# A fused attention and two-MoE kernel: order of the copies of means, the queue of the first V, and the step at which weight loads begin

## The reference, cut to what matters

```python
def _attn_ref(q, k, v):                     # B=2, H=8, S=768, D=64
    block, window = (32, 16)
    k_sum = k.reshape(B, H, nb, block, D).max(axis=3)
    v_sum = v.reshape(B, H, nb, block, D).mean(axis=3)
    scores_l = scale * q @ k^T              # kept where |i - j| < window
    scores_s = scale * q @ k_sum^T + log(block)
    a = softmax(concat[scores_l_m, scores_s])
    return a @ concat[v, v_sum]
x = transpose(attn_out).reshape(B, S, 512)
h = relu(x @ w_in);  gate = sigmoid(conv3(h, conv_w));  x = (h * gate) @ w_out
x + relu(layernorm(x) * g_ln @ w_ch1) @ w_ch2
```

## Time and profile before

| | before |
|---|---|
| median of 3 runs | 472.86 us (471.78 to 473.08) |
| profiled execution | 473.34 us, of which the span 471.60 us |
| busy: TensorE / VectorE / ScalarE / GpSimd | 457.3 / 279.9 / 200.7 / 265.9 us |
| mean granted TensorE clock | 0.996 of full speed |
| attention, steps up to 19 | until about 72 us |
| data moved by DMA | 33.61 MB in 61702 packets, 44608 of them under 512 bytes |

### The profile page before, as it was taken

The page is one execution under the profiler, slowest core; times in us unless marked ns, Lnnn a source line. Parts: engine busy times, 40 slices in busy tenths (PEclk is TensorE's granted clock), DMA queues, the critical chain, the costliest instruction groups (busy, mean ns, idle before and its releaser), DMA issues.

```text
span 471.6 us, 8651 instructions
## 1 busy us (share of the span) xinstructions
PE 457.3 (97%) x3143; PEld 404.1 (86%) x3143; DVE 279.9 (59%) x625; ACT 200.7 (43%) x499; POOL 265.9 (56%) x409
## 2 busy tenths in 40 slices
PE   6889899999999999999999999999999999999997
PEld 6667678999898998989899888989998989899985
DVE  4878896787665886894655534466652334243333
ACT  3977798533335657435423342423410331233110
POOL 3636789999905000067988778790014488788100
PEclk9998999999999999999999999999999999999999
DMA  9998872121101100001122102211020102220003
GB/s 210 195 223 201 195 182 59 46 90 45 46 0 31 60 0 1 1 0 44 47 90 89 59 33 90 89 46 44 1 111 24 61 30 89 90 72 20 0 1 133
DMA packets 61702, 33.61 MB, mean 71 GB/s; under 512 B 44608, under 2 KB 55900, under 8 KB 61660
## 3 DMA queue, kind: packets, MB, share of 16 engines
q1 hardware_dynamic: 60092, 32.66, 24.6%
q10 hardware_dynamic: 1568, 0.39, 0.4%
HBM read 28.72 MB, written 3.15 MB: 68 GB/s over the span
## 4 chain that ended last, share of the span: by engine, by line
PE 86%; SPq 8%; DVE 2%; DMA 1%; issue 1%; POOL 0%; ACT 0%; DVEq 0%; POOLq 0%
PE two L1454 9%; PE two L1455 9%; PE two L1453 9%; PE two L1430 8%; PE two L1433 8%; PE two L1432 8%; PE two L1279 5%; PE two L1281 5%; PE two L1280 5%; PE two L1359 5%; PE two L1360 5%; PE two L1358 5%; SPq L381 2%; SPq L370 2%; SPq L391 1%; PE two L1264 1%
## 5 line engine op out<-in xcount | busy, mean ns | idle before, releaser
L1430 PE MATMUL two<-combo,wa 128*128 128x384 f32 x224 | 75.9, 339 | 0.0
L1455 PE MATMUL two<-wv,h 128*128 128x512 f32 x192 | 75.4, 393 | 0.0
L1433 PE MATMUL two<-combo,wa 128*128 128x384 f32 x224 | 75.4, 336 | 0.0
L1454 PE MATMUL two<-wv,h 128*128 128x512 f32 x192 | 75.3, 392 | 0.0
L1432 PE MATMUL two<-combo,wa 128*128 128x384 f32 x224 | 75.2, 336 | 0.0
L1453 PE MATMUL two<-wv,h 128*128 128x512 f32 x192 | 75.0, 391 | 0.0
L569 POOL TENSOR_TENSOR asum<-wst 128x256 f32<-128x256 f32 x26 | 22.3, 858 | 92.4 <-PE two L1281 50.2
L598 POOL TENSOR_TENSOR wa<-wst,wa 128x256 fp32r<-128x256 f32 x39 | 29.6, 786 | 36.6 <-ACT wa L1059 36.6
L532 POOL TENSOR_SCALAR pn<-ex,rinv 128x120 f32<-128x120 f32 x96 | 33.2, 364 | 22.5 <-DVE rinv L659 22.5
L563 POOL TENSOR_TENSOR wa<-asum,wa 128x256 fp32r<-128x256 f32 x52 | 43.5, 836 | 4.3
L1279 PE MATMUL two<-xT,win 128*128 128x384 f32 x128 | 43.5, 340 | 0.0
(11 more groups left out here) (114 smaller groups left out, 984.5 us busy)
## 6 DMA issues: line engine op xcount, KB each, us to landing
wst<-in_moe_w_ch SPq DMA_DIRECT2D x26, 512.0 KB, 3.3
vW<-in_v SPq DMA_DIRECT2D x16, 240.0 KB
kn<-in_k SPq DMA_DIRECT2D x15, 192.0 KB, 3.6
qn<-in_q SPq DMA_DIRECT2D x15, 192.0 KB, 3.4
out<-y SPq DMA_DIRECT2D x11, 256.0 KB, 2.0
wst<-in_moe_w_in SPq DMA_DIRECT2D x8, 256.0 KB, 3.4
wst<-in_moe_w_out SPq DMA_DIRECT2D x8, 256.0 KB, 3.1
vW<-vs SPq DMA_DIRECT2D x16, 72.0 KB
```

The lines of the kernel that those rows point to most:

```text
L1430: nc.tensor.matmul(o, wk[:, 0, kk], ck[:, 0, kk], start=(first and kk == 0), stop=False, skip_group_check=True)
L1433: ins = nc.tensor.matmul(o, wk[:, 1, kk], ck[:, 0, kk], start=False, stop=(kk == 1), skip_group_check=True)
L1454: nc.tensor.matmul(o, hi, vl, start=False, stop=False, skip_group_check=True)
L1455: ins = nc.tensor.matmul(o, lo, vh, start=False, stop=(f == NFP - 1 and c == 1), skip_group_check=True)
```

## The change

1. SyncE no longer issues V of pair 0. ScalarE does, right after its two first loads and before its first copy of queries.
2. SyncE issues Q of pair 1 and K of pair 2 right after K of pair 1, and from pair 2 on the copies of means (`load_vsum(p)`) ahead of `load_q(p + 2)`.
3. VectorE copies the means of pair p + 1 at the end of the second step of pair p instead of in the third, and doesn't wait for outputs of step 3p any more. In exchange TensorE waits before outputs of step 3p (pairs 1 to 6) until that copy is done.
4. TensorE transposes keys of pair p + 2 before outputs of step 3p instead of after them. Scores of step 7, their maxima and their exponentials come earlier.
5. Weight splits start in step 14 instead of 9; the loads are issued at pairs 4, 5 and 6 instead of 2, 3, 5 and 6.

```diff
-        SPLIT_STEP = 9
+        SPLIT_STEP = 14
...
+        def v_parts(p):
+            b, hp = p // PPB, p % PPB
+            hh = v[b, 2 * hp:2 * hp + 2]
+            dst = vW[p % 3][:].rearrange("p n (h d) -> p n h d", h=2)
+            return [(dst[0:KEYS, 1:NQ - 1, 0], v_windows(b, 2 * hp, 1, NQ - 2, 0, KEYS)),
+                    (dst[0:KEYS, 1:NQ - 1, 1], v_windows(b, 2 * hp + 1, 1, NQ - 2, 0, KEYS)),
+                    (dst[WIN:KEYS, 0], hh[:, 0:KEYS - WIN].rearrange("h p d -> p h d")),
+                    (dst[0:KEYS - WIN, NQ - 1], hh[:, S - KEYS + WIN:S].rearrange("h p d -> p h d"))]
...
             load_k(1)
-
-            sp.wait_ge(pool_init, 1)
-            load_v(0)
             load_q(1)
             load_k(2)
+
+            sp.wait_ge(pool_init, 1)
             load_v(1)
...
+                load_vsum(p)
                 if p + 2 < NPAIR:
                     load_q(p + 2)
-                load_vsum(p)
-                for n in {2: (0,), 3: (1,), 5: (2,), 6: (3,)}.get(p, ()):
+                for n in {4: (0,), 5: (1,), 6: (2,)}.get(p, ()):
                     load_w(n)
...
-            for n in range(4, 8):
+            for n in range(3, 8):
                 load_w(n)
...
                 if p >= 2:
-                    dve.wait_ge(o_ready, GPP * (p - 1) + 1)
                     dve.wait_ge(v_in[(p - 2) % 3], v_loads(p - 2))
...
             row_sums(5)
+            score_max(7)
+            x_low(1)
             key_max(3)
+            means_out(2)
             window_keys(3)
-            x_low(1)
-            means_out(2)
...
                     row_sums(n)
+                    if p + 1 < NPAIR:
+                        means_out(p + 1)
                 elif p + 1 < NPAIR:
-                    means_out(p + 1)
                     row_sums(n)
...
             nc.scalar.dma_start(qn[:, 0, :, 1], q[0, 1].rearrange("(t p) d -> p t d", p=P)).then_inc(qn_in[0], 16)
+            act.wait_ge(pool_init, 1)
+            for dst, src in v_parts(0):
+                nc.scalar.dma_start(dst, src).then_inc(v_in[0], 16)
             queries(0, (slice(0, GB), slice(GB, NQ)))
...
+                if n % GPP == 0 and 3 <= n < GPP * (NPAIR - 1):
+                    pe.wait_ge(vm_done, p + 2)
...
             probs_t(3)
+            scores(7)
             keys_t(3)
...
                 if t == 1 and p + 1 < NPAIR:
                     block_means(p + 1)
+                    if p + 2 < NPAIR:
+                        keys_t(p + 2)
...
                 outputs(n - 1)
-                if t == 1 and p + 2 < NPAIR:
-                    keys_t(p + 2)
```

More of the change, by code:

```diff
@@ L376, in load_v @@
                     sp.wait_ge(o_ready, GPP * (p - 2))
[L377 to L384, removed]
+                for dst, src in v_parts(p):
+                    sp.dma_start(dst, src).then_inc(v_in[p % 3], 16)
             def load_vsum(p):
@@ L728, in _ @@
             row_sums(5)
+            score_max(7)
+            x_low(1)
             key_max(3)
+            means_out(2)
             window_keys(3)
-            x_low(1)
-            means_out(2)
             for n in range(6, NG):
                 p, t = n // GPP, n % GPP
-                if n + 1 < NG:
+                if 6 < n < NG - 1:
                     score_max(n + 1)
@@ L984, in _ @@
                 p, t = n // GPP, n % GPP
-                exps(n)
+                if n != 7:
+                    exps(n)
                 if n == 6:
@@ L988, in _ @@
                     x_high(2)
+                    exps(7)
                 elif t == 0:
@@ L1320, in _ @@
                     queries_t(p + 1)
-                if n + 2 < NG:
+                if 7 < n + 2 < NG:
                     scores(n + 2)
```

## The result

| | before | after |
|---|---|---|
| median, same chip, 20 executions each | 472.41 us (471.61 to 474.93) | 470.75 us (468.68 to 473.28) |
| ratio after to before | | 0.9951, 95% interval 0.9931 to 0.9972 |
| profiled execution, and its span | 473.34, 471.60 us | 470.99, 469.27 us |
| first probabilities of steps 6, 9, 12, 15, 20 | 28.02, 38.72, 47.07, 57.20, 71.73 | 28.34, 36.20, 44.53, 52.80, 69.78 |

The change makes the kernel 0.5% faster, 1.7 us by the medians and 2.3 by the ratio. The executions of the new kernel fall into two groups: nine lie between 468.68 and 469.33 us, eight between 471.09 and 473.28, three at 470.56 to 470.99. Six tenths of a per cent lie between the two groups of one and the same program, and the profiled execution, 470.99, is in the middle.

The account below looks back on a forecast made before the run. SyncE's gapless queue of issues was taken to bound the attention stage. The terms 0.4 + 4.88 - 0.6 = 4.7 us, off the median of 472.86, gave 468.2 us, with a range of 465.9 to 471.3.

Parts of the forecast that it names:

- What bounds the kernel: Attention stage, first 75 us: SyncE's gapless queue of issues makes copies late; TensorE's outputs wait 0.69 to 1.67 us.
- the transfers are the bound: Rival, attention stage: copies of pair 0 land as late as now; 471.0 us (chance 0.12) or no change, 472.9 (0.08).
- V of pair 0: Start of the kernel: pair 0's wait goes, gain 0.7 us, less 0.3 for later scores(0); net 0.4.
- SyncE is 4.4 us ahead for pair 2: SyncE's queue at pair 2: with Q's issues behind, copies may start up to 6.2 us earlier and need 1.7.
- Copies of means earlier: Attention pairs, steps 6 to 15: waits of pairs 2, 3 and 4 and the low clock go; gain 4.88 us.
- the floor: Attention pairs: VectorE, busy 7.62 of 8.36 us in one stretch, keeps a pair from going below 8.0 us.
- VectorE is no floor: Rival, attention pairs: pairs of 7.66, 7.66, 8.1 and 14.3 us, 6.7 us saved, about 466.2; chance 0.12.
- 14.53 unchanged: Stretch from step 15 to step 20: keeps its length of 14.53 us.
- Weights from step 14: Five splits move behind the attention: cost 0, as project(2) starts 4.5 us after its quarter is done.
- The new wait: Outputs of a pair's first step wait for VectorE's copy of the next means: 0.1 us at pairs 1 to 6, 0.6.
- the slower rival: Rival, pairs 1 to 6: outputs wait 1.2 us each for VectorE's copy, 7.2 paid against 5.3 gained, 474.8; chance 0.06.
- near 67: Sign that the forecast is right: step 20, from which TensorE works without a gap, starts near 67 us.

Follow-up runs that it names:

- v0_only: The kernel before with only V of pair 0 moved to ScalarE's queue, Q of pair 1 and K of pair 2 first on SyncE's; 473.42 us, ratio 1.0012.
- w_act: The changed kernel with the weight loads of pairs 4 and 5 issued by ScalarE in steps 11 and 15 instead of SyncE; 473.42 us, ratio 1.0003.
- means_only: The kernel before with only the copies of means earlier in SyncE's, VectorE's and TensorE's orders, scores(7) and maxima too; 473.08 us, ratio 1.0005.
- w_late_table: w_late plus a one-column ScalarE copy that brings the table load ahead of V of pair 0; 468.66 us (0.9907), run again 470.04 us (0.9931).
- v0_weights: The changed kernel with its means part undone, V of pair 0 on ScalarE and weights from step 14 kept; 471.64 us, ratio 0.9968.
- no_v0: The changed kernel with V of pair 0 back on SyncE, the other two parts kept; 470.32 us, ratio 0.9950.
- w_late: The changed kernel with weight splits from step 16, loads at pairs 4 and 6, the third behind all pairs; 470.99 us, ratio 0.9947.
- weights_only: The kernel before with only the weights part: splits from step 14, loads at pairs 4, 5 and 6; 470.34 us, ratio 0.9947.
- table_first: The changed kernel with only a small ScalarE copy added, so the table load is done ahead of V of pair 0; 470.93 us, ratio 0.9947.

## Why the prediction was right, and where it wasn't

The time, 470.75 us, lies in the range of 465.9 to 471.3 and is faster by more than 0.3%, as forecast. It is 2.5 us above the forecast of 468.2: 1.7 us were won of the 4.7 that the sum promised. In the profiled execution 2.3 us were won. The terms of the sum, one by one:

- **What bounds the kernel: half of it.** "Everything that comes late comes late because SyncE stands at an earlier issue" was true of the rows, and most of SyncE's time is issuing by the medians above. But it left out the two things that the runs show: V of pair 3 must wait for its buffer (`v0_only`, 1.0012), and a weight load beside V delays V itself (`w_act`, 1.0003). The rival "the transfers are the bound" (0.20 in all) gave 471.0 and came nearer to the 470.75 measured, but not for its reasons: nothing was won at the start, as it said, yet the copies of pair 0 did go 1.6 us earlier, and pair 2's clock, which it gave up, was won.
- **V of pair 0: 0.4 us gained, in the sum; -0.3 in the rows.** Step 6 came 0.32 us later. The price was sized rightly. ScalarE's timeline:

```profile
3.24 3.75 ACTq L976 DMA_DIRECT2D vW<-in_v  x4
...
7.02 1.28 ACT L924 ACT_TABLE_LOAD   x1 [7.02 <-issue]
8.31 0.86 ACT L924 COPY qT<-two 128x256 f32<-128x256 f32 x2
```

  Four issues took 3.75 us, between the bounds of 2.46 and 4.39, and scores(0) start at 8.95 in place of 8.56: 0.4 us, where 0.3 was taken. The copy starts 0.01 us after the table load ends, so the drain of 1.38 us of the Trainium skill ("ScalarE: Activation LUTs", section What ACT_TABLE_LOAD costs) isn't seen here either, and by it the start would have been about 1.8 us late (0.4 + 1.38) instead of 0.4. Pair 0's wait of 0.74 us did go, but pair 1 got 0.44 us for VectorE's copy. "SyncE is 4.4 us ahead for pair 2" failed: I followed the queue to the first wait it cures and not through the buffer that it must wait for on the way.
- **Copies of means earlier: the gain of 4.88 us from step 6 to 15 was right in size (4.72) and wrong in its cause.** The heading named "two weight loads out of the way" last of three, without a price; the terms were worked out from the order of the copies. `means_only` shows the order without that: 1.0005, and the steps of pair 4 stand 2.25 us for V. Pairs of 8.0 us came about (7.86, and 7.87 in `w_late_table`), but VectorE is busy only 6.02 of those 7.86 us and TensorE 7.76, so the reason given for the floor is not shown. The rival "VectorE is no floor" had pairs of 7.66 us; one of 7.59 stands in `v0_weights`, from step 9 to 12, right behind one of 10.86 that had waited, and none elsewhere.
- **"14.53 unchanged": the costliest error.** The stretch from step 15 to 20 became 16.98 us. Before, the copies of pair 6 were issued from 64.68 us and the outputs that need them came at 71.12. By the times of after (issued from 64.99, landed at 66.21 + 2.90 = 69.11) they had some 2.3 us to spare. TensorE was 57.20 - 52.80 = 4.40 us ahead at step 15 and the queue not at all, with a weight load right ahead of the last V; 2.1 us are missing, and 0.26 + 1.83 were waited. I had not priced how far ahead TensorE could get of a queue that stays. Nine of the 20 executions end at 469 us, close to the forecast; `no_v0`, with the same weight load ahead of its last V, has no such wait in its profile, so the load alone doesn't decide it.
- **Weights from step 14: cost 0, and no gain of its own.** The cost was right. GpSimd's timeline and the chain of waits:

```profile
100.47 0.71 POOL L543 TENSOR_SCALAR wout<-wst 128x256 fp32r<-128x256 f32 x1
101.26 1.32 POOL L545 TENSOR_TENSOR wout<-wst,wout 128x256 fp32r<-128x256 f32 x1
```

```profile
107.01 0.23 PE two L1371
```

  The 20th quarter is taken up at 100.47 us and done at 102.58, and project(2) starts at 107.01, 4.4 us later, where 4.5 were reckoned. The missing gain was the error: a term put at nothing gave 0.4 to 0.6%, 2.1 to 2.7 us, in each of four comparisons. The issues that it takes out of SyncE's queue (1.03 and 1.16 us at 31.62 and 41.56 before) are of that size as well, so this gain by itself fits issuing as much as bytes.
- **The new wait: 0.6 us charged, 0.44 seen** at pair 1 and none at pairs 2 to 5. At pair 6 it is 0.61 us where no transfer covers it (`no_v0`, `w_late`, `w_late_table`). So about 1.05 us in two places in place of 0.1 in six, and the slower rival with 1.2 us a pair never came near.

Of the signs: SyncE's gaps exist (0.50 us before 15.11, 0.75 before 23.52) but end at 24 us, where they were meant to last to 60; the clock is 1.00 through 34 to 38 us, project(2) doesn't wait, scores(0) stay below 9.4 us: as foretold. Step 20 at 69.78 lies between "near 67" and "after 70".

What stays open: how much of the third part's gain is issues, bytes or splits (splits alone don't give it, `w_act`), since no run takes bytes away and leaves the issues; what makes one execution stall at pair 4, 5 or 6 and the next not; and whether a version with weights from step 16 is faster than the change. That the slow group of executions is made of such stalls, with a lowered clock behind them, is read from the profiles at hand (those without a wait over 1 us for a transfer ran 468.70, 469.01, 469.39 and 470.46 us, those with one 470.99 to 476.14) and from the mean clock of the change's 20 executions. It wasn't tried by itself.

## What to carry to other kernels

When a queue has no gap, ask of each long issue whether it is long or held up: look at issues of the same size elsewhere (0.44 and 2.50 us here) and at what flows beside it. Sum a queue to the last consumer of the stage, buffers included, since a wait that is cured early can be paid two pairs later, clock and all (`means_only`). Keep bulk prefetch away from the transfers that the stretch waits for; another issuer didn't help here. And judge by many executions: one program gave 0.9907 in one set of six and 0.9931 in another.

## What the runs showed of the hardware that I had not expected

- **Small copies are slow.** In the 2 us in which the two copies of means of pair 6 (72 KB each, to 12 partitions) are nearly alone 60 GB/s flow (66 to 68 us); amid loads of K, Q and V it is 268 GB/s (53 to 55 us). The copies sit on TensorE's path, and being alone saves them little: the chain of waits gives the last one 2.90 us at 66.21, and 3.08 and 3.19 amid other traffic (55.99 here, 30.79 in `weights_only`).
- **Issuing a transfer of one size took from 0.44 to 2.50 us.** Both are edges of V, 40 KB each (54.63 and 61.17 in the change's profile); the smallest of V's parts had the longest issue. That what is outstanding decides it is my reading, not shown.
- **The clock is a second payment, but not always.** After waits of 1.67 us (before), 1.85 (`weights_only`), 1.87 (`v0_weights`), 2.25 (`means_only`) and 2.96 (`w_act`), and of 1.43 (`w_late`) and even of 1.19 (`table_first`), it went down to 0.50 to 0.54 of full speed in stretches of 2 us, the lower level of its two (1.2 of 2.4 GHz); after 1.83 in the change's own profile, 1.57 and 1.46 in `v0_only` and 1.53 in `v0_weights` it stayed at 1.00. The length of the last wait alone doesn't decide it.
